# A fused attention and two-FFN kernel on one core: the first two query tiles loaded as runs of four tokens, earlier in the queues, and two half scores moved between kv's last rows

## The reference

```python
def _attn_ref(q, kv, w_sr):                  # q 1 x 12288 x 128, kv 1 x 384 x 32 x 128
    kv_pool = kv.reshape(B, H // 4, 4, W // 4, 4, C).mean(axis=(2, 4))
    k = v = kv_pool.reshape(B, -1, C) @ w_sr          # 768 keys of 128
    s = (q @ k.transpose(0, 2, 1)) / np.sqrt(C)
    a = np.exp(s - s.max(-1, keepdims=True))
    a /= a.sum(-1, keepdims=True) + 1e-09
    return (a @ v).astype(np.float32)

x = _attn_ref(q, kv, w_sr)                   # 12288 x 128
h = x @ w_in1;  x = (h * (1.0 / (1.0 + np.exp(-1.702 * h)))) @ w_out1     # 128 -> 2048 -> 128
h = x @ w_in2;  out = (h * np.clip(h + 3.0, 0.0, 6.0) / 6.0) @ w_out2
```

## Time and profile before

| | |
|---|---|
| median of 3 runs | 1281.49 us (1280.74 to 1282.24) |
| time of the profiled execution | 1281.7 us |
| its span, first to last instruction | 1279.9 us |
| PE busy | 1270.7 us (99% of the span) |
| DVE, ACT busy | 1037.1 us (81%), 1035.4 us (81%) |
| POOL busy | 34.4 us (3%) |
| DMA moved | 65.69 MB, mean 51 GB/s |

### The profile page before, as it was taken

The page is one execution under the profiler, slowest core; times in us unless marked ns, Lnnn a source line. Parts: engine busy times, 40 slices in busy tenths (PEclk is TensorE's granted clock), DMA queues, the critical chain, the costliest instruction groups (busy, mean ns, idle before and its releaser), DMA issues.

```text
span 1279.9 us, 18310 instructions
## 1 busy us (share of the span) xinstructions
PE 1270.7 (99%) x5800; PEld 1055.0 (82%) x5800; DVE 1037.1 (81%) x1084; ACT 1035.4 (81%) x1216; POOL 34.4 (3%) x46
## 2 busy tenths in 40 slices
PE   8999999999999999999999999999999999999998
PEld 6888888888888888888888888888888888888887
DVE  5788888788878888888888888887888888887768
ACT  2888878888788888888888878888888888887776
POOL 1800000000000000000000000000000000000000
PEclk9999999999999999999999999999999999999999
DMA  8411311303213123032130220311303213023001
GB/s 276 129 43 41 75 45 29 74 8 66 55 18 74 28 45 74 0 74 49 25 74 12 61 62 12 74 34 40 74 0 74 49 25 74 18 48 67 1 9 17
DMA packets 183686, 65.69 MB, mean 51 GB/s; under 512 B 104561, under 2 KB 176369, under 8 KB 183409
## 3 DMA queue, kind: packets, MB, share of 16 engines
q1 hardware_dynamic: 182576, 65.30, 22.5%
q10 hardware_dynamic: 1088, 0.13, 0.1%
HBM read 22.87 MB, written 6.34 MB: 23 GB/s over the span
## 4 chain that ended last, share of the span: by engine, by line
PE 97%; SPq 1%; DMA 1%; DVE 0%; ACT 0%; issue 0%; DVEq 0%
PE pair L1081 14%; PE pair L1082 14%; PE pair L1085 14%; PE bank_av L1081 9%; PE bank_av L1085 9%; PE bank_av L1082 9%; PE bank_out L1085 7%; PE bank_out L1081 7%; PE bank_out L1082 7%; PE score_banks L1082 2%; PE score_banks L1081 2%; PE score_banks L1085 2%; DMA kv_sb<-in_kv_dram 1%; SPq L354 0%; SPq L362 0%; SPq L366 0%
## 5 line engine op out<-in xcount | busy, mean ns | idle before, releaser
L911 DVE TENSOR_TENSOR mid_lo<-work,mid_hi 128x1024 fp32r<-128x1024 f32 (+1 forms) x193 | 234.8, 1217 | 125.2 <-ACT mid_hi L628 125.1
L1081 PE MATMUL pair<-x_hi,w_hi 128*128 128x512 f32 (+1 forms) x774 | 301.1, 389 | 0.0
L1082 PE MATMUL pair<-x_hi,w_lo 128*128 128x512 f32 (+1 forms) x774 | 300.4, 388 | 0.0
L1085 PE MATMUL pair<-x_lo,w_hi 128*128 128x512 f32 (+1 forms) x774 | 300.2, 388 | 0.0
L589 ACT ACTIVATE work<-pair 128x1024 f32<-128x1024 f32 x184 | 189.4, 1029 | 119.6 <-PE pair L1085 119.5
L890 DVE TENSOR_TENSOR mid_lo<-work,mid_hi 128x1024 fp32r<-128x1024 f32 x184 | 223.5, 1214 | 25.1 <-ACT mid_hi L604 25.1
L616 ACT ACTIVATE work<-pair,half 128x1024 f32<-128x1024 f32 (+1 forms) x194 | 212.9, 1098 | 31.3 <-PE pair L1085 31.1
L903 DVE SCALAR_TENSOR_TENSOR work<-work,pair 128x1024 f32<-128x1024 f32 (+1 forms) x194 | 232.2, 1197 | 3.4 <-ACT work L616 2.7
L628 ACT ACTIVATE mid_hi<-work 128x1024 fp32r<-128x1024 f32 (+1 forms) x193 | 201.5, 1044 | 2.3 <-DVE work L903 2.3
L604 ACT ACTIVATE mid_hi<-work 128x1024 fp32r<-128x1024 f32 x184 | 194.3, 1056 | 2.2
L1081 PEld LDWEIGHTS pair<-x_hi,w_hi 128*128 128x128 f32 x774 | 145.4, 188 | 35.0 <-ACT work L589 4.2
(11 more groups left out here) (175 smaller groups left out, 1565.4 us busy)
## 6 DMA issues: line engine op xcount, KB each, us to landing
p_keys<-p_turned SPq DMA_DIRECT2D x368, 96.0 KB, 2.2
inv_b<-inv_dram SPq DMA_DIRECT2D x23, 256.0 KB, 3.3
out_dram<-y_sb SPq DMA_DIRECT2D x92, 64.0 KB, 2.5
q_raw<-in_q_dram SPq DMA_DIRECT2D x88, 64.0 KB, 2.0
kv_sb<-in_kv_dram SPq DMA_DIRECT2D x6, 768.0 KB, 9.7
w_raw<-in_moe_w_in_dram SPq DMA_DIRECT2D x2, 1024.0 KB, 7.5
kv_sb<-in_kv_dram SPq DMA_DIRECT2D x6, 256.0 KB, 8.1
inv_dram<-inv_t SPq DMA_DIRECT2D x92, 0.5 KB
```

The source lines that it names most:

```text
L911: dve.tensor_tensor(in_pair(mid_lo[mid2(t, p)], t, p, c), in_pair(act2[p % 2], t, p, c), in_pair(mid_hi[mid2(t, p)], t, p, c), ALU.subtrac ...
L1081: pe.matmul(dst, a_hi, b_hi, start=start, stop=False)
L1082: pe.matmul(dst, a_lo, b_hi, start=False, stop=False)
L1085: return pe.matmul(dst, a_hi, b_lo, start=False, stop=stop)
```

## The change

Tile 0's queries are loaded behind kv's second group instead of its sixth, and each SBUF partition now takes four consecutive tokens, one contiguous run of 2 KB, instead of four rows of 512 bytes. A slot of the turned queries then holds every fourth token, so the instructions that read them from PSUM put them back into token order: they read with a stride of 128 elements inside groups of four (`from_fours`) and write four neighbours (`in_fours`). Tile 1's queries are four DMAs of the same kind, behind kv's last row in SP's queue with no wait before them.

PE turns tile 0's queries behind kv's second group, tile 1's before slot 0's second half. ACT makes tile 0's high part first of all, DVE its low part behind kv's third group. Slots 1 and 2 are scored on the first 384 keys between kv's rows. The first values move to the other bank of `pair2`, and DVE makes their low part before the last three rows.

```diff
-    q_first = q[:, 0:TILE].rearrange("b (s p) c -> p (b s) c", p=128)
-    q_second = q[:, TILE:2 * TILE].rearrange("b (a s i) c -> i (b a) s c", a=4, i=32)
+    q_first = q[:, 0:TILE].rearrange("b (p j) c -> p (b j c)", j=4)
+    q_second = q[:, TILE:2 * TILE].rearrange("b (a s i j) c -> s a i (b j c)", a=4, s=4, j=4)
...
-        VALUES_IN = [pair[2][:, 0:HALF], bank_out[:, 0:HALF]]
+        VALUES_IN = [pair[2][:, 512:512 + HALF], bank_out[:, 0:HALF]]
         Q_FIRST_IN = [bank_out[:, :], pair[2][:, 512:1024]]
+
+        def in_fours(ap):
+
+            return ap.rearrange("c (p j) -> c p j", j=4)
+
+        def from_fours(ap):
+
+            return ap.rearrange("c (j p) -> c p j", j=4)
...
-                    if g == KV_GROUPS - ROW_GROUPS - 1:
+                    if g == 1:
                         load_q_first()
...
-            sp.wait_ge(kv_row_loaded[ROW_GROUPS - 1][0], 16)
-            for a in range(4):
-                sp.dma_start(q_raw1[32 * a:32 * (a + 1), :].rearrange("p (s c) -> p s c", s=SLOTS),
-                             q_second[:, a]).then_inc(q1_loaded, 16)
+            for n in range(4):
+                sp.dma_start(q_raw1[32 * n:32 * (n + 1), :], q_second[n]).then_inc(q1_loaded, 16)
...
-                act.activation(q_hi[:, :], Q_FIRST_IN[0], ACT.Copy, scale=SCALE).then_inc(q_hi_ready, 1)
+                act.activation(in_fours(q_hi[:, :]), from_fours(Q_FIRST_IN[0]), ACT.Copy,
+                               scale=SCALE).then_inc(q_hi_ready, 1)
...
-                act.activation(q_t[:, :], Q_FIRST_IN[1], ACT.Copy, scale=SCALE).then_inc(q1_copied, 1)
+                act.activation(in_fours(q_t[:, :]), from_fours(Q_FIRST_IN[1]), ACT.Copy,
+                               scale=SCALE).then_inc(q1_copied, 1)
...
+            q_high_first()
             pooled_copy(0)
             k_hi_copy(0)
-            q_high_first()
             v_hi_copy(0)
...
-                dve.scalar_tensor_tensor(out=q_lo[:, :], in0=Q_FIRST_IN[0], scalar=SCALE, in1=q_hi[:, :],
-                                         op0=ALU.mult, op1=ALU.subtract).then_inc(q_lo_ready, 1)
+                dve.scalar_tensor_tensor(out=in_fours(q_lo[:, :]), in0=from_fours(Q_FIRST_IN[0]), scalar=SCALE,
+                                         in1=in_fours(q_hi[:, :]), op0=ALU.mult,
+                                         op1=ALU.subtract).then_inc(q_lo_ready, 1)
...
             for g in range(KV_GROUPS - ROW_GROUPS):
                 add_pixels(g)
+                if g == 2:
+                    q_low_first()
             k_lo_part(0)
             add_row_pixels(KV_GROUPS - 2, 0)
             add_row_pixels(KV_GROUPS - 2, 1)
-            q_low_first()
             add_row_pixels(KV_GROUPS - 2, 2)
+            v_lo_part(0)
             add_row_pixels(KV_GROUPS - 1, 0)
             add_row_pixels(KV_GROUPS - 1, 1)
             add_row_pixels(KV_GROUPS - 1, 2)
-            v_lo_part(0)
...
-            for g in range(1, 4):
+            pool_group(1)
+            keep_busy(3, rows=2)
+            turn_q_first(0)
+            for g in range(2, 4):
                 pool_group(g)
                 keep_busy(3 if g < 3 else 1, rows=2)
             pe.wait_ge(w_sr_loaded, 16)
             keys_of(0)
             pool_group(4)
             values_of(0)
-            turn_q_first(0)
             pool_group(5)
...
             scores_half(0, 0, 0)
             pool_loaded_row(6, 2)
-            for a in range(KV_ROWS):
-                pool_loaded_row(7, a)
+            scores_half(0, 1, 0)
+            pool_loaded_row(7, 0)
+            scores_half(0, 2, 0)
+            pool_loaded_row(7, 1)
+            pool_loaded_row(7, 2)
             keys_of(1)
             keys_of(2)
             values_of(1)
+            pe.wait_ge(v_lo_ready, 1)
+            turn_q_first(1)
 
             pe.wait_ge(k_hi_ready, PARTS)
             scores_half(0, 0, 1, low=(k_lo_ready, PARTS)).then_inc(scores_ready, 1)
-            turn_q_first(1)
-            scores_half(0, 1, 0)
             scores_half(0, 1, 1).then_inc(scores_ready, 1)
-            pe.wait_ge(v_lo_ready, 1)
-            scores_half(0, 2, 0)
             pe.wait_ge(q1_copied, 1)
             scores_half(0, 2, 1).then_inc(scores_ready, 1)
```

More of the change, by code:

```diff
@@ L347, in load_q_first @@
             def load_q_first():
-                sp.dma_start(q_raw[:, :].rearrange("p (s c) -> p s c", s=SLOTS), q_first).then_inc(q0_loaded, 16)
+                sp.dma_start(q_raw[:, :], q_first).then_inc(q0_loaded, 16)
             for g in range(KV_GROUPS):
```

## The result

| | before | after |
|---|---|---|
| median of the runs on one chip | 1281.30 us (1280.74 to 1282.24, 22 runs) | 1283.28 us (1282.87 to 1285.10, 22 runs) |
| profiled execution, its span | 1281.7, 1279.9 us | 1283.6, 1281.8 us |

The changed kernel takes **1.98 us longer**, a ratio of 1.0018 (95% interval 1.0012 to 1.0024). That is slower by less than 0.2%, but the interval does not hold a ratio of 1. It lies 0.3 above the predicted 1283.0.

The account below looks back on a forecast made before the run. The prologue up to tile 1's first scores at 31.67 us sets the end, PE being full afterwards. 0.69 + 1.04 - 0.1 + 0.47 - 0.6 = 1.5 us gave 1283.0, range 1281.2 to 1284.2.

Parts of the forecast that it names:

- Where the end is set: Prologue before 31.67 us: PE is full afterwards, so any shift of tile 1's first scores shifts the end equally.
- Tile 0's load, 0.69: Load ahead of four whole kv groups: 256 KB delay groups 2 to 5 by 0.69 us, bounds nothing to 0.9.
- DVE's list: DVE before kv's sixth group: queries' low part (0.68) and 0.60 wait fit in 1.5 us idle, about 0.3 left.
- PE among the rows, 1.04 less 0.1 of waits: PE from sixth group's passes to last keys: full, so two half scores add 1.04, less 0.1; keys at 25.38.
- Behind the keys: Last keys to second maximum: transposes add 0.47, 0.6 comes back; second maximum at 29.43, 1.49 later.
- The turn's 0.47: Tile 1's four transposes, now ahead of slot 0's last product on PE, add 0.47 us.
- Strided reads: Reordering reads of PSUM on ACT and DVE: no cost taken, 0.60 to 0.70 each; bounds no cost to twice the time.
- rival B: Strided reads, k times a contiguous one, stall DVE's intake of kv; slower by over 0.2%, 1285.1 at k = 3; 10 in 100.
- the prediction's estimate: By the skill's rule on non-contiguous PSUM reads: strided reads at least twice as long, time 1283.9.
- Tile 1's load: Four DMAs without a wait land soon behind kv's last row, over 2 us before needed at 26.80; counted at nothing.
- 0.81 for all the rest: Terms besides tile 0's load: half scores 1.04, less 0.1 waiting, plus 0.47 transposes, less 0.6 coming back.
- The case's own range: 1282.1 to 1283.8: load's shift 0.3 to 0.9, a half score 0.35 to 0.59, DVE 0.3 us late.

Follow-up runs that it names:

- Experiment 9: Runs of four without the wait, plus tile 1's turn behind both halves of slot 1 and ACT's copy behind the first exponential: 1282.12 us, ratio 1.0007.
- experiment 2: Changed kernel with tile 0's load, turn, high and low part back at their old places behind kv's sixth group: 1282.21 us, ratio 1.0007.
- experiment 3: Kernel before with runs of four, no wait, and tile 0's load alone moved behind kv's second group: 1282.34 us, against 1281.30 without that move.
- experiment 5: Changed kernel with tile 0's load behind kv's third group instead of its second: 1282.67 us, ratio 1.0015.
- experiment 1: Changed kernel with the first halves of slots 1 and 2 put back behind slot 0's second half: 1282.50 us, ratio 1.0009.
- experiment 4: Changed kernel with tile 1's turn put back behind slot 0's second half: 1282.98 us, ratio 1.0015.
- experiment 6: Kernel before with runs of four and the reordering reads alone, the wait ahead of tile 1's load kept: 1284.60 us, ratio 1.0022.
- experiment 7: Kernel before with runs of four and without the wait ahead of tile 1's load: 1280.86 us, ratio 0.9998; its repeat 1281.30 us.

## Why the prediction was right, and where a term was off

**Where the end is set.** "Whatever the prologue does to the moment at which PE starts tile 1's first scores, the end does too": 2.12 there, 1.96 in the span. From tile 1's first scores to the row of `x_hi` and `ones` it takes PE 5.88 before (31.67 to 37.55) and 5.88 in the changed kernel. Experiment 9 shows the bound of the sentence: there it takes 6.29, because of a late split by POOL.

**Tile 0's load, 0.69: this is the term that was too small.** It is 1.07 by experiment 2 and 1.04 by experiment 3, and 0.69 lies outside what resampling allows either. The reason given for it, 256 KB at the pace of kv's own groups, is right: the step behind the second group is 2.66 on average with the load in it (four profiles, 2.62 to 2.69) and 1.99 without (eight, 1.95 to 2.04), so 0.67. The rest, 0.4, was not foreseen: the bounds, nothing to 0.9, let only the queries' own bytes cost something, not the group ahead of them. The second group itself came at 10.34 on average where queries are queued right behind it (four profiles) and at 10.02 where they are not (eight). The first of these spreads from 9.53 to 10.97 and the second from 9.39 to 10.84, so this 0.32 is only suggested by the profiles, though experiments 3 and 5 point the same way. The trace has each engine's share of a DMA landing by itself. The second group's sixteen shares land from 7.47 to 10.33 in the changed kernel, and DVE starts at 10.36: it waits for the slowest engine. On average over the shares the second group is only 0.1 later with queries behind it (8.76 against 8.65). What makes up the remaining 0.4 stays open.

**DVE's list.** It was said that the low part fits in DVE's idle time ahead of groups 3 to 5 with 0.3 left. It was closer than that: the prediction's own terms, 1.5 less 0.68 and 0.60, leave 0.2. And PE had turned the queries so late that DVE waited 0.73 for the high part and took the fourth group at 15.94 with no wait for DMA. It caught up at the sixth group, with a wait of 0.20 left. But the pooling of that group then found PE still with the keys and values of part 0, and began at 21.17, 2.03 behind the group instead of 1.61: 0.42 that no step had. About 0.1 of it is the change's, since the early low part holds back the fourth group and with it PE's keys: the three other profiles with the early turn begin 1.70 to 1.74 behind. The other 0.3 is this profile's alone, and goes back to PE's clock. Timeline of PE in the changed kernel, eight matmuls on constants that keep it busy while it waits for kv:

```profile
8.82 3.76 PE L1179 MATMUL pair<-patch,ident 128*128 128x288 f32 x8
12.42 0.80 PE L1104 MATMUL pair<-patch,kv_sb 128*128 128x96 f32 x6
```

And in the kernel before:

```profile
8.55 2.13 PE L1169 MATMUL pair<-patch,ident 128*128 128x288 f32 x8
11.50 0.91 PE L1094 MATMUL pair<-patch,kv_sb 128*128 128x96 f32 x6 [0.82 <-DVE kv_sb L774]
```

The same eight take 3.76 instead of 2.13, and the second group, on DVE only 0.46 later, is pooled 0.92 later. The constant matmuls start 0.48 apart up to 12.1 us here; in the kernel before they start 0.48 apart up to 7 us and 0.24 apart from 8.8 on. The trace's list of clock changes begins with full clock at 12.11 here and at 8.26 there. So PE was at the lower of its two levels, 1.2 GHz, for almost 4 us longer, and turned tile 0's queries late for that reason.

**PE among the rows, 1.04 less 0.1 of waits.** The file was said to take 5.15 from the sixth group's passes to the keys and took 4.88, since it started later and so met no late row at all: 0.27 better. The half scores cost 0.93 in the file (experiment 1). By experiment 2, whose pooling starts on time, they cost 1.01 (19.46 to 24.68, against the old 4.21). With 0.52 more at the landing of the sixth group (19.14 against 18.62), 0.42 at PE's start and 0.27 less in the file, the keys came at 26.05 instead of 25.38.

**Behind the keys.** From the keys to the second maximum 4.05 was forecast (25.38 to 29.43) and 4.01 measured; the slot that counted was slot 1's and is now set by DVE's own list, as said. The turn's 0.47 costs 0.36 by experiment 4.

**What was counted at nothing.** Strided reads cost nothing (0.60 and 0.69), so rival B, with its DVE stalled by k times as long a read, has no case. The Trainium skill, page "SBUF — State Buffer", section "Door 1: The DMA port swizzle", says that such patterns slow matmuls; by the prediction's estimate they would have taken twice as long at least if that held for ACT and DVE, and in this trace it does not. Tile 1's load was covered, too: its last share landed at 24.42, 3.1 before PE turned it at 27.55. But how much hung on it was not seen. In the kernel before, the same load with the wait kept cost 3.3 (experiment 6), where nothing had been expected.

**Sum.** Forecast: 0.69 for the load, 0.81 for all the rest, 1.5. By medians: 1.04 for the load (experiment 3) and 0.94 for the rest (experiment 2), 1.98 in all. The profile pair shows 1.21 at the sixth group and 0.91 behind it. The first is larger than the medians bear out, as one profile's start can be, and the second has about 0.2 of the late clock in it; experiment 2 without that has 0.81 (14.55 less 13.74). The time came out inside the range with one term a third too small. The case's own range, given as 1282.1 to 1283.8, comes out of its stated bounds as 1282.3 to 1283.7.

## What to carry to other kernels

Work put "into the gaps" of a stream is free only on an engine that has gaps. PE's rows take 0.45 each and arrive 0.6 apart, which looks like room, but PE was already behind when they came: compare the end of all its work so far with the arrival of the last piece, not one piece with one interval. A load moved ahead in a stream costs its bytes to everyone behind it, and the group right ahead may pay as well; move it only if what needs it would otherwise wait, and here nothing had waited for tile 0's queries. When a transfer's place and its shape change together, test them apart: taking the wait away alone cost 0.7, the runs of four alone 3.3, and both together nothing. Before a profile is read to tenths of a us, look where its first DMAs landed and when PE's clock rose: both differ from one execution to the next.

## What the hardware showed that was not expected

- **One DMA shape, two prices.** Four DMAs of 32 partitions with 2 KB each, issued from 21.20 on by a queue that waited for the first row of kv's last group, fed PE only at 28.47; issued from 14.36 on, behind the rows in the queue, they had landed by 24.67. In pieces of 512 bytes the late issue was fine (turn at 26.20) and the early one held up kv by 0.9.
- **The long runs are carried by four engines.** The trace lists every step of a DMA's semaphore. For tile 1's four DMAs there are 64 steps with the old layout, one for each of 16 engines and DMA, and 20 with the runs of four. In the changed kernel four of the 20 come at 14.96 to 17.07, just behind the issues and long before kv's last row is there (23.06), so they are not data. The other 16 come in fours, 22.29 to 22.50, 22.94 to 23.15, 23.58 to 23.79 and 24.22 to 24.42: four engines with 16 KB each for a DMA, 0.64 for a share. In experiment 6 the first three DMAs landed by 25.83 and half of the fourth by 26.57; its last two shares came at 27.97 and 28.42, while the first of the weights, 1024 KB issued at 24.14, was moving too. Why those two came so late stays open.
- **DMA starts slowly, and one engine sets the pace.** From 5 to 8 us the queues move 228 to 288 GB/s in the twelve profiles, with or without the change, and 373 to 408 from 11 to 14 us. In the repeat of experiment 7, by stretch (the last number is GB/s):

```profile
5.00:8.00 3.00, 2.69 (x8) 1.58 (x6) 1.52 (x2) 0.00 (x0) 0.00 (x0) 1.00 0.96 258
8.00:11.00 3.00, 2.67 (x13) 1.90 (x12) 0.85 (x1) 0.00 (x0) 0.00 (x0) 1.00 1.00 350
11.00:14.00 3.00, 2.14 (x14) 1.85 (x15) 2.19 (x4) 0.00 (x0) 0.00 (x0) 1.00 1.05 406
```

  The engines are busy, yet carry less. The sixteen shares of the second group land 1.5 to 3.5 us apart, and DVE must wait for the last of them. An engine that is behind stays behind: in the changed kernel the shares of the third group lie 2.15 apart, those of the sixth 2.14 and those of kv's last row 2.04. So the moment of the second group's arrival varies from 9.39 to 10.97, and shifts a whole profile by over 1 us. Single profiles of these kernels must be compared from that group on.
- **PE's clock rises at a different time in each execution.** The first clock change in the trace, to full, comes at 5.83 to 8.75 us in eleven profiles and at 12.11 in the changed kernel's. Ahead of it the constant matmuls of 288 columns start 0.48 apart, behind it 0.24. The view by stretch shows a granted clock of 1.00 for the time ahead of the first change, too, as in the first row above; the steps of the matmuls tell the truth there.
